# Linear attention ahead of a mixture of experts: the attention loop rewritten with row and column tiles on TensorE, scores one chunk ahead, and loads that don't wait for stores

## The chip, the cores and the metric

The kernel runs on one core of a Trainium2 chip. It is one program with five engines: TensorE (PE, its weight loads are shown as PEld), VectorE (DVE), ScalarE (ACT), GpSimd (POOL) and SyncE (SP), which here only issues DMAs. The metric is the device time of one execution in microseconds (us), lower is better.

## What is computed

```python
for t in range(S):                                   # B, H, S, D = 2, 8, 768, 48
    kt, vt, rt = (k[:, :, t], v[:, :, t], r[:, :, t])
    cur = np.einsum('bhd,bhe->bhde', u[None] * kt, vt)
    y[:, :, t] = np.einsum('bhd,bhde->bhe', rt, state + cur)
    state = w[None, :, :, None] * state + np.einsum('bhd,bhe->bhde', kt, vt)
x = y as (1536 tokens, 384)
logits = x @ w_gate                                  # 8 experts, the best one takes the token
...                                                  # each expert keeps its first 384 tokens
out[i] = gate[i] * (relu(x[i] @ w1[e]) @ w2[e])
g = relu(out @ w_in) ** 2                            # d_ff 2048
result = g @ w_out
```

Here w is a decay per head and feature, u a bonus that the token gives to itself.

## The kernel before, in words

**Stages.** First the attention, in chunks of 128 tokens; then routing (which token goes to which expert) and the gather of the tokens' rows from DRAM; then eight experts with four pieces of weights each and an MLP over the tokens in three blocks of 512, with eight pieces each. The experts and the MLP use f32r matmuls on values that are split into a high and a low part (whi and wlo, xshi and xslo), which the change does not touch.

**The attention loop.** There are 12 chunks: 6 along the sequence for each of 2 batches, taken in turn, so that chunk n belongs to batch n % 2. The loop runs 3 times over 4 slots (`for u in range(SLOTS)`), and slot u has its own input buffers. Heads lie in pairs (g of 4): the even head's 48 features stand in partitions 0 to 47, the odd head's in 64 to 111 (ROWS = 112). Within a chunk the recurrence is three products: scores of the chunk's keys against its queries, masked so that only earlier tokens count; the queries against the state before the chunk; and the bonus of each token with itself. Powers of w come from a table T made at the start (L746 to L769); keys and queries are scaled with them.

- SP (L279 to L312): loads feat (queries and keys by feature), vT, rk (queries and keys by token) and vx for the first four chunks and two pieces of expert weights; then for each chunk n it waits for x of n, issues its store to DRAM, waits until that store has landed (`x_stored`, L306), and only then issues the four loads of chunk n + 4. The wait for the landing is there because the buffers of slot u are reused.
- POOL (L360 to L373): scales keys (L364) and queries (L365), then khat (keys by token, for the state, L371) and ru (queries times u by token, L373).
- ACT (L620 to L641): copies the scaled keys into Kb, where each head has zeros in the other head's rows; copies v times gate from PSUM into vx; copies vx into vb, again with zeros; and scales the state St into Sd in four instructions (L640).
- PE (L414 to L447): v times gate (L421), scores (L427), the new state's product (L435), then for each head pair the state's part (L443) and the masked scores' part (L445) of y. Each f32 matmul is carried out as two instructions, a transpose as one. All of them use the whole array, 128 or 112 stationary columns.
- DVE (L784 to L811): masks the scores in two halves (L790), multiplies ru by the keys (L794) and sums over features (csum, L795), multiplies vx by csum (cv, L797), adds cv to y (x_sb L800 and heads_l L801), adds the new product to the state (L806, two instructions) and sums the heads' parts of the gate logits into L (L809).

DVE, ACT and PE take the chunks in order, and each of them does a chunk's steps in the order of the list. y of chunk n needs the masked scores and the state after chunk n - 2.

**After the loop.** DVE works out from L which token goes where (from L830), PE counts (L452 to L461), POOL gathers the first expert's rows from DRAM (L384), PE turns them (L513) and the first hidden matmuls begin (L477). Pieces 2 and 3 of the weights are issued behind the last loads of the loop, pieces 4 to 7 as soon as the lo part of pieces 0 to 3 has been split off (L313 to L315).

Of the kernel before, what the change touches and what calls it, by code (L numbers as in the profile page):

```python
# [20 lines left out]
P = 128  # L21
F32 = mybir.dt.float32
# [4 lines left out]
ALU = mybir.AluOpType  # L27
# [29 lines left out]
CONSTS = 10  # L57
SLOTS = 4

def build(nc, feat_d, vT_d, rk_d, vx_d, w_d, u_d, wg_d, wts_d, xd, out):
    with ExitStack() as ctx:
# [47 lines left out]
        with ExitStack() as a:  # L110
            feat = [sb(f"feat{u}", [P, 2, G * C], F32, a) for u in range(SLOTS)]
            rk = [sb(f"rk{u}", [P, 2, DM], F32, a) for u in range(SLOTS)]
            vx = [sb(f"vx{u}", [P, H, DX], F32, a) for u in range(SLOTS)]
            vT = [sb(f"vT{u}", [P, KT, C], F32, a) for u in range(SLOTS)]
            Rd = [sb(f"Rd{u}", [P, G * C], F32, a) for u in range(SLOTS)]
            Kb = [sb(f"Kb{u}", [P, G, 2, C], F32, a) for u in range(2)]
            vb = [sb(f"vb{u}", [P, G, 2, 2 * DX], F32, a) for u in range(2)]
            khat = [sb(f"khat{u}", [P, G, P], F32, a) for u in range(SLOTS)]
            ru = [sb(f"ru{u}", [P, DM], F32, a) for u in range(SLOTS)]
            x_sb = [sb(f"x_sb{u}", [P, DM], F32, a) for u in range(SLOTS)]  # L120
            am = sb("am", [P, 2, G * C], F32, a)
            csum = sb("csum", [P, H], F32, a)
            cv = sb("cv", [P, H, DX], F32, a)
            heads_l = sb("heads_l", [P, H, E], F32, a)
            St = [sb(f"St{b}", [P, G, 2 * DX], F32, a) for b in range(B)]
            Sd = sb("Sd", [P, G, 2 * DX], F32, a)
            T = sb("T", [P, G, 256], F32, a)
            Tk = sb("Tk", [P, G, C], F32, a)
            Tr = sb("Tr", [P, G, C], F32, a)
            iw = sb("iw", [P, G], F32, a)  # L130
            wcol = sb("wcol", [P, G], F32, a)
            tokw = sb("tokw", [P, G, P], F32, a)
            ub = sb("ub", [P, DM], F32, a)
# [12 lines left out]
        bank = [ctx.enter_context(nc.psum_tensor(f"bank{j}", [P, 512], F32)) for j in range(8)]  # L146
        ps_a0, ps_a1, ps_y, ps_kv, ps_x, ps_pos, ps_tab, ps_tab2 = bank
        ps_a = [ps_a0, ps_a1]
# [23 lines left out]
        tr_ready = sem("tr_ready")  # L172
        tokw_psum = sem("tokw_psum")
        tokw_ready = sem("tokw_ready")

        k_decayed = sem("k_decayed")
        r_decayed = sem("r_decayed")
        kb_cleared = sem("kb_cleared")
        kb_ready = sem("kb_ready")
        sd_ready = sem("sd_ready")  # L180
        khat_ready = sem("khat_ready")
        ru_ready = sem("ru_ready")
        khat_cleared = sem("khat_cleared")
        vb_cleared = sem("vb_cleared")
        vb_ready = sem("vb_ready")
        scored = sem("scored")
        masked = sem("masked")
        kv_done = sem("kv_done")
# [870 lines left out]
```

## Time and profile before

| | us |
|---|---|
| median of 3 runs (lowest, highest) | 481.53 (480.67, 483.12) |
| the profiled execution | 486.22 |
| its span, first to last instruction | 484.5 |
| PE busy, whole span | 437.6 (90%) |
| DVE busy | 300.9 (62%) |
| ACT busy | 219.9 (45%) |
| POOL busy | 112.2 (23%) |

The profile is of one execution. Busy time of PE is modelled from instructions that overlap one another, so a busy PE isn't PE at its peak; where the text needs the price of a matmul it takes the step from one to the next out of the chain of waits. L12 is line 12 of the kernel. In an instruction's shape, 128\*112 is the stationary operand, and 128x112 behind it the moving one. "<-" behind an idle time names what ended it.

### The profile page before, as it was taken

The numbers are of one execution on the slowest core, as the hardware profiler recorded it, in microseconds if no ns is written. First come the engines' busy times: TensorE is split into PE (matmuls) and PEld (weight loads), VectorE is DVE, ScalarE is ACT, GpSimd is POOL, SyncE is SP. The second block draws the span as 40 slices with busy tenths as digits, with TensorE's granted clock in tenths as the row PEclk, the third lists the DMA queues.
The fourth block names the chain that finished last, engine by engine and source line by source line (L and its number), as shares of the span: only waits on it lengthen the run. The fifth ranks groups of instructions, "written<-read, shape, count | busy, mean of one in ns | idle before, by whom it ended". The sixth has DMA issues, their size and how long they took to land.

```text
span 484.5 us, 8560 instructions
## 1 busy us (share of the span) xinstructions
PE 437.6 (90%) x2922; PEld 412.2 (85%) x2923; DVE 300.9 (62%) x494; ACT 219.9 (45%) x382; POOL 112.2 (23%) x110
## 2 busy tenths in 40 slices
PE   3998988723979999999999999999999999999993
PEld 3997978612979999999999989899898989899892
DVE  8797989883564677577676385454645545454431
ACT  3453544511454555565565364444544444444320
POOL 6855765528620220210000000000300000300003
PEclk9998999965898999999999999999999999999997
DMA  8966676504593555654555523232431313400001
GB/s 205 277 235 199 188 222 197 210 22 171 169 391 107 193 185 171 218 171 179 195 159 170 197 66 129 67 102 95 126 134 65 130 65 129 133 0 0 1 0 65
DMA packets 20990, 69.50 MB, mean 143 GB/s; under 512 B 3353, under 2 KB 9770, under 8 KB 20961
## 3 DMA queue, kind: packets, MB, share of 16 engines
q1 hardware_dynamic: 18656, 64.40, 41.2%
q0 software_dynamic: 2304, 4.73, 2.7%
q8 instruction: 17, 0.28, 0.2%
q14 instruction: 13, 0.10, 0.1%
HBM read 64.39 MB, written 7.08 MB: 148 GB/s over the span
## 4 chain that ended last, share of the span: by engine, by line
PE 76%; DVE 13%; issue 6%; DMA 2%; DVEq 1%; POOL 0%; ACT 0%; POOLq 0%; ACTq 0%
PE bank L477 34%; PE bank L496 21%; PE bank L486 14%; DVE cv L797 3%; DVE ru L794 2%; PE bank L445 2%; DMA xg<-attention_out,gidx 2%; PE bank L468 1%; DVE am L790 1%; DVE St L806 1%; PE bank L427 1%; PE bank L443 1%; DVE csum L795 1%; PE bank L435 1%; DVE L L809 1%
## 5 line engine op out<-in xcount | busy, mean ns | idle before, releaser
L908 DVE TENSOR_TENSOR wlo<-raw,whi 128x1536 fp32r<-128x1536 f32 x56 | 98.4, 1758 | 100.3 <-ACT whi L615 100.3
L615 ACT ACTIVATE whi<-raw 128x1536 fp32r<-128x1536 f32 x56 | 83.2, 1488 | 87.5 <-PE bank L496 47.1
L397 POOL DMA_INDIRECT out<-osb,oidx x12 | 13.0, 1084 | 247.7 <-ACT osb L730 245.3
L496 PE MATMUL bank<-whi,hhi 128*128 128x384 f32 x192 | 64.9, 338 | 0.5 <-DVE hlo L927 0.5
L496 PE MATMUL bank<-wlo,hhi 128*128 128x384 f32 x192 | 64.8, 338 | 0.0
L496 PE MATMUL bank<-whi,hlo 128*128 128x384 f32 x192 | 64.8, 338 | 0.0
L477 PE MATMUL bank<-xshi,whi 128*128 128x256 f32 x192 | 57.0, 297 | 5.0 <-issue 3.3
L477 PE MATMUL bank<-yhi,whi 128*128 (+1 forms) x144 | 57.1, 396 | 0.0
L477 PE MATMUL bank<-yhi,wlo 128*128 (+1 forms) x144 | 57.0, 396 | 0.0
L477 PE MATMUL bank<-ylo,whi 128*128 (+1 forms) x144 | 56.6, 393 | 0.0
L486 PE MATMUL bank<-hhi,whi 128*128 128x256 f32 x192 | 55.9, 291 | 0.0
L477 PE MATMUL bank<-xshi,wlo 128*128 128x256 f32 x192 | 55.7, 290 | 0.0
L477 PE MATMUL bank<-xslo,whi 128*128 128x256 f32 x192 | 55.6, 289 | 0.0
L486 PE MATMUL bank<-hhi,wlo 128*128 128x256 f32 x192 | 54.2, 282 | 0.0
L486 PE MATMUL bank<-hlo,whi 128*128 128x256 f32 x192 | 53.9, 281 | 0.0
L669 ACT ACTIVATE rl<-bank 128x512 f32<-128x512 f32 x48 | 28.6, 600 | 54.6 <-PE bank L477 51.1
L923 DVE TENSOR_TENSOR sq<-rl 128x512 f32<-128x512 f32 x48 | 32.9, 690 | 30.1 <-ACT rl L669 30.1
L384 POOL DMA_INDIRECT xg<-attention_out,gidx x24 | 27.7, 1156 | 91.4 <-PE bank L468 71.3
L477 PEld LDWEIGHTS bank<-xshi,whi 128*128 128x128 f32 x192 | 37.9, 197 | 6.3 <-issue 3.7
L477 PEld LDWEIGHTS bank<-xslo,whi 128*128 128x128 f32 x192 | 38.2, 199 | 0.0
L496 PEld LDWEIGHTS bank<-whi,hhi 128*128 128x128 f32 x192 | 36.1, 188 | 1.9 <-issue 0.9
L477 PEld LDWEIGHTS bank<-xshi,wlo 128*128 128x128 f32 x192 | 37.7, 196 | 0.0
(155 smaller groups left out, 848.8 us busy)
## 6 DMA issues: line engine op xcount, KB each, us to landing
raw<-in_wts SPq DMA_DIRECT2D x56, 768.0 KB, 4.7
feat<-in_feat SPq DMA_DIRECT2D x12, 448.0 KB, 4.0
rk<-in_rk SPq DMA_DIRECT2D x12, 384.0 KB, 4.6
vx<-in_vx SPq DMA_DIRECT2D x12, 224.0 KB, 5.1
vT<-in_vT SPq DMA_DIRECT2D x12, 192.0 KB, 3.8
attention_out<-x_sb SPq DMA_DIRECT2D x12, 192.0 KB, 4.9
out<-rl SPq DMA_DIRECT2D x12, 192.0 KB
xg<-attention_out,gidx POOLq DMA_INDIRECT x24, 5.9
```

The source lines that it names most:

```text
L384: nc.gpsimd.indirect_dma_start(out=xg[e % 2][:, q, :], out_offset=None, in_=xd[:, :], in_offset=bass.IndirectOffsetOnAxis(ap=gidx[:, e * C ...
L397: nc.gpsimd.indirect_dma_start(out=out[:, :], out_offset=bass.IndirectOffsetOnAxis(ap=oidx[:, t:t + 1], axis=0), in_=osb[:, t, :], in_offs ...
L445: mm = pe.matmul(pair, am[:, g // 2, (2 * (g % 2) + o) * C:(2 * (g % 2) + o + 1) * C], vb[u % 2][:, g, o, :], start=False, stop=(o == 1))
L477: mm = pe.matmul(banks[ft][:, 0:width], w[:, r, cols], x(k), start=(k == 0 and step == 0), stop=(k == KT - 1 and step == 2))
L486: mm = pe.matmul(ps_e[dt][:, 0:width], w[:, r, cols], x[:, par, ft, 0:width], start=(q == 0 and ft == 0 and step == 0), stop=(q == EQ - 1 ...
L496: mm = pe.matmul(ps_o[tt][:, 0:DM], x[:, par, ft, tt * P:(tt + 1) * P], w[:, r, cols], start=(v == 0 and ft == 0 and step == 0), stop=(v = ...
L615: return nc.scalar.activation(dst, src, ACT.Copy)
L669: nc.scalar.activation(rl[:, ft, :], banks[ft][:, :], ACT.Relu).then_inc(h_relu, 1)
L794: after(v.tensor_tensor(ru[u][:, :], ru[u][:, :], rk[u][:, 1, :], ALU.mult))
L797: after(v.tensor_tensor(cv[:, :, :], vx[u][:, :, :], csum[:, :].unsqueeze(2).to_broadcast([P, H, DX]), ALU.mult))
L908: v.tensor_tensor(wlo[:, r, :], raw[:, r, :], whi[:, r, :].bitcast(F32), ALU.subtract).then_inc(w_lo, 1)
L923: v.tensor_tensor(sq[:, ft, :], rl[:, ft, :], rl[:, ft, :], ALU.mult).then_inc(h_sq, 1)
```

## The change

- SP: chunk 0 is loaded ahead of the gate weights. The load of chunk n + 4 waits for x of chunk n to be summed, then the store of chunk n is issued once ACT has copied it; nothing waits for a landing but ACT, before it writes the same x_sb buffer four chunks later. rk is no longer loaded. Weight pieces 0 to 3 are issued behind the stores of chunks 1, 3, 5 and 7; pieces 4 to 7 wait for the three first gathers.
- POOL: keys and queries are scaled in place; khat and ru go.
- PE: `scores(n + 1)` (v times gate, the keys turned by four transposes, the scores) runs before the rest of chunk n. The stationary operand is cut in halves of 64 columns (column tiles, at output partitions 0 and 64) for v times gate, csum, the state's product and y; scores and the state's part of y use 48 rows at partition 0 or 64 (row tiles), so that no zeros are needed. The bonus is a matmul of prod (queries times keys) with a two-column operand (csum). Matmuls with 56 moving columns take the place of 112 wide ones.
- ACT: copies the turned keys to kT and the v times gate part to vx, scales the state in four instructions, copies x to x_sb. Kb, vb and Sd go.
- DVE: prod, one mask instruction 1024 wide, cv (its factor csum now in PSUM), Sn (the state's sum), yx (y plus cv, both parts in one), L. ru, csum, heads_l go.
- The loop of PE and DVE runs twice and the last four chunks are written out; those of ACT and SP are written out wholly. The power table is half as long, some constants and clearings go, and v and the gate weights lie in another head order.

```diff
...
+            sp.dma_start(ucol[0:ROWS, :], u_d).then_inc(in_u, 16)
             sp.dma_start(wg[:, :, :], wg_d).then_inc(in_wg, 16)
-            for u in range(SLOTS):
+            for u in range(1, SLOTS):
                 load_chunk(0, u)
-                if u == 0:
-                    sp.dma_start(ub[:, :], u_d.partition_broadcast(P)).then_inc(in_u, 16)
-            load_weights(0, 0)
-            load_weights(1, 1)
-            with sp.Fori(1, NC_ // 2) as i:
+            for i in range(1, NC_ // 2 + 1):
                 for u in range(SLOTS):
-                    sp.wait_ge(x_ready, 4 * (i - 1) + u + 2)
+                    n = 4 * (i - 1) + u
+                    if i < NC_ // 2:
+                        sp.wait_ge(x_ready, n + 2)
+                        load_chunk(i, u)
+                    sp.wait_ge(x_copied, n + 3)
                     store_x(i - 1, u)
-                    sp.wait_ge(x_stored[u], 16 * i)
-                    load_chunk(i, u)
-            load_weights(2, 2)
-            load_weights(3, 3)
-            for u in range(SLOTS):
-                sp.wait_ge(x_ready, NT - SLOTS + u + 2)
-                store_x(NC_ // 2 - 1, u)
+                    if n % 2 and n < 2 * RING:
+                        load_weights(n // 2, n // 2)
+            for q in range(CT):
+                sp.wait_ge(first_gathered[q], 16)
...
-                    keys = chunk_view(feat[u][0:ROWS, 1, :])
-                    nc.gpsimd.tensor_tensor(keys, keys, Tk[0:ROWS, :, :], ALU.mult).then_inc(k_decayed, 1)
-                    nc.gpsimd.tensor_tensor(chunk_view(Rd[u][0:ROWS, :]), chunk_view(feat[u][0:ROWS, 0, :]),
+                    nc.gpsimd.tensor_tensor(chunk_view(feat[u][0:ROWS, 1, :]), chunk_view(feat[u][0:ROWS, 1, :]),
+                                            Tk[0:ROWS, :, :], ALU.mult).then_inc(k_decayed, 1)
+                    nc.gpsimd.tensor_tensor(chunk_view(feat[u][0:ROWS, 0, :]), chunk_view(feat[u][0:ROWS, 0, :]),
                                             T[0:ROWS, :, 0:C], ALU.mult).then_inc(r_decayed, 1)
-                    pool.wait_ge(in_tok[u], 32 * (i + 1))
-                    pool.wait_ge(tokw_ready, 1)
-                    pool.wait_ge(khat_cleared, SLOTS if u else 1)
-                    pool.wait_ge(in_u, 16)
-                    nc.gpsimd.tensor_tensor(gapped(khat[u][:, :, :]), pairs(rk[u][:, 1, :]),
-                                            gapped(tokw[:, :, :]), ALU.mult).then_inc(khat_ready, 1)
-                    nc.gpsimd.tensor_tensor(ru[u][:, :], rk[u][:, 0, :], ub[:, :], ALU.mult).then_inc(ru_ready, 1)
...
+            def scores(i, u):
+
+                n = 4 * i + u
+                pe.wait_ge(in_vT[u], 16 * (i + 1))
+                for k in range(KT):
+                    for half in halves:
+                        pe.matmul(ps_vwg[half, 0:H * E], vT[u][:, k, half], wg[:, k, :], start=(k == 0), stop=(k == KT - 1))
+                pe.wait_ge(k_decayed, n + 1)
+                for g in range(G):
+                    mm = pe.transpose(ps_kT[:, g * ROWS:(g + 1) * ROWS], feat[u][0:ROWS, 1, g * C:(g + 1) * C], ident[0:ROWS, 0:ROWS])
+                mm.then_inc(turned, 1)
+                pe.wait_ge(r_decayed, n + 1)
+                for g in range(G):
+                    for o, rows in enumerate(heads):
+                        mm = pe.matmul(score_banks[:, o, g * C:(g + 1) * C], feat[u][rows, 1, g * C:(g + 1) * C],
+                                       feat[u][rows, 0, g * C:(g + 1) * C], start=True, stop=True)
+                mm.then_inc(scored, 1)
+
+            def attend(i, u, last):
+
+                n, p, b = 4 * i + u, u % 2, u % 2
+                pe.wait_ge(vx_ready, n + 1)
+                if not last:
+                    pe.wait_ge(masked, n + 1)
+                    if u < SLOTS - 1:
+                        scores(i, u + 1)
+                    else:
+                        scores(i + 1, 0)
+                pe.wait_ge(prod_ready, n + 1)
+                pe.wait_ge(summed, n + 1)
+                for g in range(G):
+                    for half in halves:
+                        pe.matmul(ps_csum[half, 0:H].rearrange("p (o g) -> p g o", o=2)[:, g, :],
+                                  prod[p][0:ROWS, g * C + half.start:g * C + half.stop], bonus[0:ROWS, g, :], start=True, stop=True)
+                pe.wait_ge(x_ready, n + 1)
+                pe.wait_ge(state_ready, 4 * n + 4)
+                for g in range(G):
+                    for o, width in enumerate((HALF, D)):
+                        mm = pe.matmul(ps_kv[ODD * o:ODD * o + width, g * DX:(g + 1) * DX], kT[p][:, g, ODD * o:ODD * o + width],
+                                       vx[u][:, o * G + g, :], start=True, stop=True)
+                mm.then_inc(kv_done, 1)
+                for g in range(G):
+                    pair = slice(g * DX, (g + 1) * DX)
+                    for half in halves:
+                        for o, rows in enumerate(heads):
+                            mm = pe.matmul(y_banks[half, o, pair], feat[u][rows, 0, g * C + half.start:g * C + half.stop],
+                                           St[b][rows, g, :], start=True, stop=False)
+                    if g == G - 1:
+                        mm.then_inc(state_read, 1)
+                    if g == 0:
+                        pe.wait_ge(masked, n + 1)
+                    for o in range(2):
+                        for half in halves:
+                            mm = pe.matmul(y_banks[half, o, pair], am[p][:, o * G + g, half], vx[u][:, o * G + g, :],
+                                           start=False, stop=True)
+                mm.then_inc(y_done, 1)
...
+            def columns(i, u):
+
+                n = 4 * i + u
+                act.wait_ge(turned, n + 1)
+                copy(kT[u % 2][:, :, :].rearrange("p g r -> p (g r)"), ps_kT[:, 0:G * ROWS]).then_inc(kT_ready, 1)
+                act.wait_ge(in_tok[u], 16 * (i + 1))
+                copy(vx[u][:, :, D:DX], ps_vwg[:, 0:H * E].rearrange("p (h e) -> p h e", h=H)).then_inc(vx_ready, 1)
+
+            def advance(i, u, last):
+
+                n, b = 4 * i + u, u % 2
+                if not last:
+                    if u < SLOTS - 1:
+                        columns(i, u + 1)
+                    else:
+                        columns(i + 1, 0)
+                act.wait_ge(summed, n + 2)
+                act.wait_ge(state_read, n + 1)
+                for g in range(G):
+                    nc.scalar.activation(St[b][0:ROWS, g, :], Sn[b][0:ROWS, g, :], ACT.Copy,
+                                         scale=T[0:ROWS, g, 129:130]).then_inc(state_ready, 1)
+                act.wait_ge(x_ready, n + 2)
+                if i:
+                    act.wait_ge(x_stored[u], 16 * i)
+                copy(x_sb[u][:, :].rearrange("p (g o d) -> p o g d", g=G, o=2),
+                     yx[u % 2][:, :, 0:D].rearrange("p (o g) d -> p o g d", o=2)).then_inc(x_copied, 1)
...
+            def weigh(i, u):
+
+                n, p = 4 * i + u, u % 2
+                dve.wait_ge(r_decayed, n + 1)
+                v.tensor_tensor(prod[p][w, :], feat[u][w, 0, :], feat[u][w, 1, :], ALU.mult).then_inc(prod_ready, 1)
+                dve.wait_ge(scored, n + 1)
+                v.tensor_tensor(am[p][:, :, :], score_banks[:, :, :].rearrange("p o (g s) -> p (o g) s", g=G),
+                                before[:, :].unsqueeze(1).to_broadcast([P, H, C]), ALU.mult).then_inc(masked, 1)
+
+            def collect(i, u, last):
+
+                n, p, b = 4 * i + u, u % 2, u % 2
+                if not last:
+                    if u < SLOTS - 1:
+                        weigh(i, u + 1)
+                    else:
+                        weigh(i + 1, 0)
+                dve.wait_ge(kv_done, n + 1)
+                after(v.tensor_tensor(cv[:, :, :], vx[u][:, :, :], ps_csum[:, 0:H].unsqueeze(2).to_broadcast([P, H, DX]), ALU.mult))
+                dve.wait_ge(state_ready, 4 * n + 4)
+                v.tensor_tensor(Sn[b][w, :, :], ps_kv[w, 0:G * DX].rearrange("p (g e) -> p g e", g=G), St[b][w, :, :],
+                                ALU.add).then_inc(summed, 1)
+                dve.wait_ge(y_done, n + 1)
+                dve.wait_ge(x_copied, n + 1)
+                v.tensor_tensor(yx[p][:, :, :].rearrange("p (o g) d -> p o (g d)", o=2), y_banks[:, :, 0:G * DX],
+                                cv[:, :, :].rearrange("p (o g) d -> p o (g d)", o=2), ALU.add).then_inc(x_ready, 1)
+                dve.wait_ge(x_ready, n + 2)
+                after(v.tensor_reduce(L[:, bass.ds(n, 1), :].rearrange("p a e -> p (a e)"),
+                                      yx[p][:, :, D:DX].rearrange("p h e -> p e h"), AX.X, ALU.add))
...
```

## Rows read from the trace of the kernel before

**Rows 1.** Stages: length; busy us of PE, PEld, DVE, ACT, POOL; clock, DMA, GB/s

```profile
...
20.00:32.00 12.00, 12.00 (x112) 12.00 (x111) 10.97 (x21) 6.51 (x19) 7.98 (x7) 1.00 0.79 258
32.00:98.00 66.00, 55.71 (x469) 53.73 (x467) 57.89 (x92) 30.83 (x78) 40.35 (x34) 0.97 0.65 206
...
```

**Rows 2.** Chain that ended last: start, us; the first scores, then one chunk

```profile
10.51 3.52 PE bank L427 x16
...
46.41 0.63 PE bank L421 x6
47.04 1.84 PE bank L427 x16
48.88 0.79 PE bank L435 x8
...
49.88 0.45 PE bank L445 x4
...
```

**Rows 3.** Waits of the queue of SP: total us, times, longest

```profile
SPq L281 <- DMA attention_out<-x_sb: 41.0, 8, 9.7
...
```

**Rows 4.** Instructions in time, SP's queue: start, us, what

```profile
...
36.59 0.33 SPq L281 DMA_DIRECT2D feat<-in_feat  x1
...
38.74 0.36 SPq L289 DMA_DIRECT2D attention_out<-x_sb  x1
...
```

**Rows 5.** DMA issues of the page: times, KB each, median us to landing

```profile
feat<-in_feat SPq DMA_DIRECT2D x12, 448.0 KB, 4.0
...
attention_out<-x_sb SPq DMA_DIRECT2D x12, 192.0 KB, 4.9
...
```

**Rows 6.** Groups by shape, 0 to 125 us: busy, mean ns | idle before

```profile
...
L364 POOL TENSOR_TENSOR feat<-feat,Tk 112x512 f32<-112x512 f32 x12 | 15.7, 1305 | 23.0 <-DMA feat<-in_feat 23.0
L790 DVE TENSOR_TENSOR am<-bank,before 128x512 f32<-128x512 f32 x24 | 15.6, 687 | 3.4 <-DVE L L809 1.1 <-PE bank L427 1.0
...
```

**Rows 7.** Instructions in time, 51 to 60 us, DVE and POOL

```profile
...
51.56 0.63 DVE L797 TENSOR_TENSOR cv<-vx,csum 128x448 f32<-128x448 f32 x1
...
57.82 2.83 DVE L797 TENSOR_TENSOR cv<-vx,csum 128x448 f32<-128x448 f32 x1
...
59.16 1.00 POOL L373 TENSOR_TENSOR ru<-rk,ub 128x384 f32<-128x384 f32 x1
...
```

**Rows 8.** Instructions in time: POOL's first, a quiet ru, weights behind routing

```profile
...
7.22 1.27 POOL L364 TENSOR_TENSOR feat<-feat,Tk 112x512 f32<-112x512 f32 x1 [1.98 <-DMA feat<-in_feat]
...
93.16 0.55 DVE L794 TENSOR_TENSOR ru<-ru,rk 128x384 f32<-128x384 f32 x1
...
107.46 2.97 SPq L292 DMA_DIRECT2D raw<-in_wts  x2
...
```

**Rows 9.** The same chain: gaps of DVE, then routing, gather and a turn

```profile
38.65 0.42 issue
...
39.83 0.40 DVE St L806
...
97.87 0.26 DVE r_mx L830
...
99.56 0.55 PE bank L454 x12
...
105.24 0.68 issue
...
108.83 7.42 DMA xg<-attention_out,gidx
...
149.07 0.33 PE bank L468 x3
...
```

**Rows 10.** Groups by shape, PE: 128 or 112 stationary columns, 112 moving

```profile
L445 PE MATMUL bank<-vb,am 128*128 128x112 f32 x192 | 30.4, 283 | 0.0
...
L435 PE MATMUL bank<-vx,khat 128*112 128x112 f32 x96 | 12.4, 276 | 7.0 <-DVE St L806 7.0
...
```

More of the change, by code:

```diff
@@ L57, with build @@
 CONSTS = 10
+HALF = P // 2
 SLOTS = 4
-def build(nc, feat_d, vT_d, rk_d, vx_d, w_d, u_d, wg_d, wts_d, xd, out):
+def build(nc, feat_d, vT_d, vx_d, w_d, u_d, wg_d, wts_d, xd, out):
     with ExitStack() as ctx:
@@ L188, in build @@
         kv_done = sem("kv_done")
+        summed = sem("summed")
+        state_read = sem("state_read")
         state_ready = sem("state_ready")
@@ L191, in build @@
         x_ready = sem("x_ready")
-        vwg_psum = sem("vwg_psum")
-        vx_ready = sem("vx_ready")
+        x_copied = sem("x_copied")
         shifted = sem("shifted")
@@ L404, in _ @@
         def _(pe):
+            halves = [slice(0, HALF), slice(HALF, P)]
+            heads = [slice(0, D), slice(ODD, ROWS)]
+            def scores(i, u):
[14 more added lines that the diff above has]
+                mm.then_inc(scored, 1)
@@ L449, in _ @@
+                    attend(i, u, False)
+            for u in range(SLOTS):
+                attend(NC_ // 2 - 1, u, u == SLOTS - 1)
             pe.wait_ge(oh_ready, 1)
@@ L643, in split_hi @@
+            columns(0, 0)
+            for i in range(NC_ // 2):
+                for u in range(SLOTS):
+                    advance(i, u, 4 * i + u == NT - 1)
             def split_hi(m, r, turns):
@@ L746, in _ @@
             v.memset(T[w, :, 64:65], 1.0)
[L747 to L748 removed]
+            v.memset(oh[:, :, :], 0.0)
             dve.wait_ge(in_w, 16)
@@ L775, in _ @@
-            v.memset(x_sb[SLOTS - 1][:, :], 0.0).then_inc(x_ready, 1)
-            for u in range(1, SLOTS):
-                v.memset(khat[u][:, :, :], 0.0).then_inc(khat_cleared, 1)
+            v.tensor_copy(Tk[w, :, :], T[w, :, 127::-1]).then_inc(table_ready, 1)
+            v.tensor_tensor(T[w, :, 129], T[w, :, 128], T[w, :, 128], ALU.mult)
+            after(v.memset(bonus[w, :, :], 0.0))
+            dve.wait_ge(in_u, 16)
+            for o in range(2):
+                rows = slice(ODD * o, ODD * o + D)
+                v.tensor_tensor(bonus[rows, :, o], ucol[rows, :], wcol[rows, :], ALU.mult).then_inc(bonus_ready, 1)
@@ new lines, in _ @@
+            v.memset(Sn[0][:, :, :], 0.0).then_inc(summed, 1)
+            for b in range(B):
+                v.memset(St[b][:, :, :], 0.0).then_inc(state_ready, 4)
+            v.memset(start[:, :], 0.0).then_inc(x_ready, 1)
+            v.memset(kept[:, :], 0.0).then_inc(x_copied, 2)
+            dve.wait_ge(consts, 2)
+            def weigh(i, u):
[5 more added lines that the diff above has]
+                                before[:, :].unsqueeze(1).to_broadcast([P, H, C]), ALU.mult).then_inc(masked, 1)
@@ L778, in _ @@
+            weigh(0, 0)
+            with dve.Fori(0, NC_ // 2 - 1) as i:
+                steps.enter(i, 2 * SLOTS)
+                for u in range(SLOTS):
+                    collect(i, u, False)
+                steps.leave(NC_ // 2 - 1)
+            for u in range(SLOTS):
+                collect(NC_ // 2 - 1, u, u == SLOTS - 1)
             v.memset(gout[:, :], 0.0).then_inc(y_ready, 1)
```

176 lines of the change are left out of this document (35 added, 141 removed).

## The prediction

> **What bounds the kernel now.** I read the stages first. The attention loop fills the span from 8.5 to 98 us, then come some 21 us of routing and gather, then 365 us of expert and MLP matmuls, where the page shows PE busy nine tenths or more in nearly every slice. Only the first stage is rewritten, so the question is what ends one chunk (12 chunks, one batch's 128 tokens each) and how the next stage starts. In the loop the stages have two paces. From 20 to 32 us PE is busy for all 12 of 12 us, and the steps of a chunk add up to 0.63 + 1.84 + 0.79 + 4 x 0.67 = 5.9 us [rows 1, 2]; from 32 to 98 us PE is busy 84% and DVE 88% [rows 1]. The reader should not stop at the engine with the largest share: the queue that issues DMAs shows why the pace falls. SP waits 41.0 us in 8 waits for a store of x_sb to land, before it may issue the next loads [rows 3]. Its cycle is four loads, from 36.59 to 38.74 2.15 us, then a store, which lands 4.9 us after its issue [rows 4, 5], and some 0.2 us of waking: 7.3 us a chunk. Behind it POOL waits for feat, 23.0 us in all [rows 6], and everything follows. The bunching has a second effect: cv on DVE, with two inputs in SBUF, takes 0.63 us in one chunk and 2.83 us in the next, where it ends (60.65) only after POOL's operation from 59.16 to 60.16 has ended [rows 7]. So three limits stand close together: SP's order 7.3 us, DVE with its waits some 7 us, PE 5.9 us.
>
> **SP.** The loads of chunk n+4 no longer wait for the store of chunk n to land; they need that x(n) is summed. One load of four (rk, 384 KB) goes. SP then issues three loads and a store a chunk at 0.54 us each, 2.2 us [rows 4]; the 768 KB weight pieces move from before the loop to behind chunks 1, 3, 5 and 7, 0.5 us each. Queued behind SP's wait for x_copied are the next loads; that copy comes only some 0.7 us after x is summed (an ACT copy of 0.5, a wait of 0.2, by ACT's tokw copy of 0.54 us), so this costs nothing. Is a load early enough? From x(n) to the matmuls that need chunk n+4: 0.5 us issue, 4.0 us landing [rows 5], 2.6 us on POOL (2 x 1.305 [rows 6]), 7.1 us; two chunks at 6 us, less 0.8, give 11.2. It stays hidden down to a chunk of 4 us. Volume: 448+192+224+192 KB and, in the first eight, 384 KB of weights, 1.44 MB in 6 us, 240 GB/s, where 258 GB/s were moved from 20 to 32 us at a DMA share of 0.79, so up to some 325 [rows 1]. This is the thinnest cover of the three; if it tears, feat is late as now.
>
> **DVE.** Gone per chunk: ru, csum, heads_l and the second St; cv takes its factor from PSUM, so it has one SBUF input. Left or new: prod 512 wide, 0.55 x 512/384 = 0.73 from the ru at 93.16, when POOL is quiet [rows 8]; am 1024 wide, two of 0.687 less an overlap, 1.29 [rows 6]; cv 0.63 [rows 7]; Sn 0.40 as one St [rows 9]; yx 448 wide, as cv, 0.63; L 0.27 as before: 3.95 us. A gap between dependent steps is up to 0.42 us [rows 9]; six at half of that give 1.2. That is 5.15, and up to 2.2 more if prod meets POOL as cv did; I take 5.3.
>
> **ACT and POOL.** ACT is busy 30.83 of 66 us [rows 1], 3.4 us a chunk; it loses Kb and vb (four copies) and gets kT and the copy of x (two, 0.5 each), so it does less than now. POOL keeps 2.6 us and loses khat and ru. Neither is near 6 us.
>
> **PE, the term that decides.** Every f32 matmul is two instructions, a transpose one. Before, a chunk has 6+16+8+8+16 = 54. After: 12 for v times gate, 4 transposes, 16 scores, 16 csum, 16 kv, 64 for y (16 state and 16 am matmuls), 128 in all. What does one cost? The step is 0.45/4 = 0.112 us with 128 stationary columns and 112 moving, 0.115 with 128 and 128, 0.105 with 128 and 64, but 0.79/8 = 0.099 with 112 and 112 [rows 2, 10]. The moving width hardly counts and the stationary one does (0.099/0.112 = 0.88, 112/128 = 0.875). So a half of 64 columns should cost 0.056. Whether two tiles in different halves run side by side no row shows, since before has none. Upper end, not at all: 108 x 0.056 + 4 x 0.11 (0.33 for 3 [rows 9]) + 16 x 0.112 = 8.3 us. Lower end, all in pairs: 108 x 0.028 + 0.44 + 0.9 = 4.4 us. A chunk may thus cost PE less or more than the present 5.9. I take 6.0, a little below the middle (6.35), because the order written in the change alternates halves from matmul to matmul, for which only the shortest seen step speaks as a floor: bf16 steps of 0.55/12 = 0.046 us [rows 9]. 108 x 0.042 + 0.44 + 0.9 = 5.9, and 0.1 for waits.
> The rule most in favour is in the Trainium skill, "TensorE: Matmul & The Clock Gate", Part 3 (packing small matmuls): matmuls of different row or column tiles run at once. By that alone the sum is that of the lower end; no run here shows it yet.
>
> **What orders a chunk after.** PE does scores(n+1), then csum, kv and y of n. am(n+1) is made while kv and y(n) run (2.4 us of DVE work beside over 4 us of PE work), and kv(n) waits for yx(n-1), some 0.9 us after y(n-1), which lies beside scores (1.9 us). So the masks leave the path, and the longer engine's sum sets the pace: PE 6.0, DVE next at 5.3. Two waits are new. ACT waits for the store of four chunks ago before it copies x; the next kT and vx stand behind it, but that store has some 20 us for its 4.9. PE waits for the mask of n before scores(n+1), one PSUM pair only, with all of chunk n behind it; the mask is made 2.5 us after the scores, beside kv and y of n-1, so it is ready.
>
> **The start and the rest.** The first feat load is issued one place earlier, about half a microsecond, as wg moves behind chunk 0. POOL began at 7.22 [rows 8]; so keys are ready at 8.0 and queries at 9.3. Scores at the start ran at half pace (3.52 us for 16 against 1.84 [rows 2]): 1.8 us in pairs, and am with its wait 1.5: 12.6, I say 12.8. Of twelve chunks the last has no scores to make (v times gate 0.5, 0.44, 0.9). A slow first chunk 1.5, the last yx and L 1.3. L is complete at 12.8 + 72 - 1.85 + 1.5 + 1.3 = 85.8 us, against 97.87 [rows 9]: 12.1 us gained. The constants, tokw and zeroing that go lay beside POOL's wait: nothing.
> From L to gidx the code is the same. The stores: the last x is copied 0.5 us later and lands 4.9 us after [rows 5], while the indices take 7.4 us (97.87 to 105.24 [rows 9]): hidden, 2 us to spare. The gathers: SP now holds back the weight pieces 4 to 6 until the first three have landed; before, two pieces went out from 107.46 on [rows 8], beside the 7.42 us for which the chain waits for the gather [rows 9]. POOL's own work of issuing fills part of that time, so I give it 1.0 us, between 0 and 2. The held pieces then come some 9 us later, 7 to 9 us for 2.3 MB, while the first four pieces are in SBUF and are worked through first; I cost it at nothing, and at up to 3 us if that cover is short. The 365 us behind are not touched.
>
> **Sum.** 12.1 + 1.0 = 13.1 us. The profiled execution took 486.22 us (span 484.5), so 473.1; it was 4.7 us above the median of the runs, which I subtract: 468.4 us.
>
> **The rivals.**
> - Tiles pair fully and DVE is the bound. PE 4.4, DVE 5.3: 0.7 us x 12 = 8.4 less, 460.0 us. For: the order of the matmuls. Against: nothing below 0.046 a step is seen.
> - Slower: each change between full, row-split and column-split use empties the array. A matmul lasts 0.283 us [rows 10] while the next starts after 0.112 [rows 2]; the tail is 0.17. Per chunk the form changes 3 times before csum and 8 times in kv and y, where state and am alternate by head pair: 11 x 0.17 = 1.9 us, x 12 = 22.4, 490.8 us. It decides from about 0.10 us a change, where a chunk passes 7.1 us. Before has no such change, so the trace is silent. Beside it: the Trainium skill, "TensorEngine Tiling (Array Packing)", Key Properties, says that a change of tiling mode drains the engine.
> - Slower as well: halves don't pair at all, 8.3 us, 27.6 more, 496 us.
> - It moves nothing: prod, the one operation with two SBUF inputs, meets POOL each time as cv did (2.2 us longer), DVE needs 7.3, the pace of now. Gain left from the start alone: 12 x 1.3 = 15.6 less gain, 484.0 us. For: POOL has work all the time once loads run free. Against: POOL is busy 2.55 of 6 us only. Loads that come late through the added weight traffic would give the same time.
>
> **How the numbers follow.** Forecast 0.46, pairs fully 0.22, array emptied 0.13 (half of the price in a third of these cases, near 480), not paired 0.05, nothing moved 0.14. A measurement of this kernel can tell about 0.5%, 2.4 us. Faster: 0.46 + 0.22 and some of the nothing-moved and half-price cases, 0.75; same 0.08; slower 0.17. Range 456 to 491: down past the DVE bound by the doubt of the start and gather terms (4 us), up to the emptied array; only the unpaired case and tails are out.
>
> **What would show it.** Right: SP has no wait for the landing of a store; POOL's waits for feat are short; from 20 us on PE is the busy engine and chunks come every 6 us; the groups for csum, kv and y have a spacing near 0.04 us; L complete near 86 us. Wrong: a y stage of over 3.5 us a chunk (tiles not paired, or gaps at each change of form); prod over 1.5 us; feat landing after 6 us; a granted clock of a half in the loop; or a gap at the first weight pieces behind the gather, which would show as a wait for wlo after 119 us.

## The result and the profile after

The changed kernel takes 507.88 us (median of 4 runs, 506.29 to 509.43), the kernel before, run beside it, 482.32 us (480.67 to 483.82). The ratio is 1.0546, with a 95% interval from 1.0493 to 1.0599: 25.6 us slower. The profiled execution has a span of 504.6 us, against 484.5.

The loop ends later and the rest is shorter. L is complete (the start of r_mx) at 124.75 us, before at 97.87 [rows 9]: 26.9 us later. From there to the end it is 379.9 us, before 386.6: 6.8 us less. The sum is the 20.1 us between the spans.

First the stretches: length, then busy us of PE, PEld, DVE, ACT and POOL, the granted clock, the DMA share and GB/s (the counterpart of [rows 1]).

```profile
...
20.00:50.00 30.00, 30.00 (x408) 25.38 (x408) 11.49 (x18) 6.66 (x21) 7.49 (x6) 1.00 0.43 136
50.00:80.00 30.00, 30.00 (x410) 25.49 (x404) 12.01 (x19) 7.70 (x25) 7.48 (x6) 1.00 0.49 161
...
```

PE is busy in all of the time, up to 110 us too, and nothing else is near it: DVE 40%, the DMAs under half. So nothing waits that matters. The chain that ended last shows one chunk (start, us, what), the counterpart of [rows 2]:

```profile
60.29 0.65 PE bank L391 x12
60.95 0.94 PE bank L394 x4
61.89 2.01 PE score_banks L399 x16
63.90 0.95 PE bank L417 x16
64.85 0.94 PE bank L423 x14
65.78 0.41 PE y_banks L430 x8
66.19 0.61 PE y_banks L438 x8
...
```

The two causes of waiting in the kernel before are gone. SP has no wait for a landed store left (41.0 us in [rows 3]). POOL's wait for feat has grown, from 23.0 [rows 6] to 59.3 us, against what the prediction named as a sign of being right, and it costs nothing: it is idle time of an engine that is ahead. Waits of 20 to 110 us (engine, line, waited for: total us, times, longest), then SP's:

```profile
POOL feat L346 <- DMA feat<-in_feat: 59.3, 8, 9.7
DVE yx L809 <- PE y_banks L438: 29.5, 10, 3.0
...
SPq L267 <- DVE yx L809: 68.0, 8, 14.9
SPq L274 <- ACT x_sb L617: 31.9, 4, 9.2
```

### The profile page after: what moved, and what is told of

Read it like the earlier page. It is cut to its first block, busy times and chain, and to the rows that moved or that the text cites. A ratio compares the mean times of both kernels' runs of the same rounds, so it can differ in the third digit from the quotient of the medians.

```text
span 504.6 us, 9950 instructions
## 1 busy us (share of the span) xinstructions
PE 471.9 (94%) x3806; PEld 431.0 (85%) x3807; DVE 268.4 (53%) x442; ACT 205.5 (41%) x357; POOL 84.2 (17%) x85
## 4 chain that ended last, share of the span: by engine, by line
PE 90%; DVE 3%; issue 2%; DMA 2%; DVEq 1%; POOL 0%; SPq 0%; ACT 0%; POOLq 0%; ACTq 0%
PE score_banks L479 17%; PE bank L479 15%; PE y_banks L498 10%; PE bank L498 10%; PE y_banks L488 9%; PE y_banks L438 6%; PE score_banks L399 5%; PE bank L488 4%; PE y_banks L430 4%; PE bank L423 2%; PE bank L394 2%; PE bank L417 2%; PE bank L391 2%; PE bank L470 1%; DMA xg<-attention_out,gidx 1%
## 5 line engine op out<-in xcount | busy, mean ns | idle before, releaser
L488 PE MATMUL y_banks<-hhi,whi 128*128 128x256 f32 x128 | 37.8, 296 | 0.0
L488 PE MATMUL y_banks<-hhi,wlo 128*128 128x256 f32 x128 | 36.1, 282 | 0.0
L488 PE MATMUL y_banks<-hlo,whi 128*128 128x256 f32 x128 | 36.0, 281 | 0.0
L498 PE MATMUL y_banks<-whi,hhi 128*128 128x384 f32 x96 | 32.5, 338 | 0.5 <-DVE hlo L942 0.5
L438 PE MATMUL y_banks<-vx,am 128*64 128x56 f32 x384 | 32.6, 323 | 0.0
L498 PE MATMUL y_banks<-whi,hlo 128*128 128x384 f32 x96 | 32.4, 338 | 0.0
L498 PE MATMUL y_banks<-wlo,hhi 128*128 128x384 f32 x96 | 32.4, 338 | 0.0
L498 PE MATMUL bank<-whi,hhi 128*128 128x384 f32 x96 | 32.4, 338 | 0.0
L498 PE MATMUL bank<-wlo,hhi 128*128 128x384 f32 x96 | 32.4, 338 | 0.0
L498 PE MATMUL bank<-whi,hlo 128*128 128x384 f32 x96 | 32.4, 338 | 0.0
```

What stands on the lines that cost most here:

```text
L438: mm = pe.matmul(y_banks[half, o, pair], am[p][:, o * G + g, half], vx[u][:, o * G + g, :], start=False, stop=True)
L488: mm = pe.matmul(ps_e[dt][:, 0:width], w[:, r, cols], x[:, par, ft, 0:width], start=(q == 0 and ft == 0 and step == 0), stop=(q == EQ - 1 ...
L498: mm = pe.matmul(ps_o[tt][:, 0:DM], x[:, par, ft, tt * P:(tt + 1) * P], w[:, r, cols], start=(v == 0 and ft == 0 and step == 0), stop=(v = ...
```

## The experiments

Two theories stood after the result. One: changes between full array, row tiles and column tiles are dear, and half matmuls hardly pair. Two: they pair, and the pattern of matmuls keeps the clock at its lower level. Wherever a diff is not against the kernel after, the text says so.

**e1: the freed loads by themselves** (diff against the kernel before).

```diff
                     store_x(i - 1, u)
-                    sp.wait_ge(x_stored[u], 16 * i)
                     load_chunk(i, u)
...
                     dve.wait_ge(y_done, n + 1)
+                    dve.wait_ge(x_stored[u], 16 * i + 1)
```

> The kernel before with one part of the change: the loads of chunk n+4 no longer wait for the store of chunk n to land (VectorE waits for that before it writes the same x_sb buffer). If the order of SP's queue set the 7.3 us pace from 32 to 98 us, nine chunks fall to the next bound, TensorE's 5.9 us or VectorE's 6.4 us with its gaps: 0.8 to 1.3 us each, 7 to 12 us in all, 470 to 475 us. If VectorE held behind GpSimd (cv up to 2.83 us) set the pace by itself, the time stays within 2 us of 482.

477.15 us (474.16 to 479.28, 10 runs), ratio 0.9893 (0.9856 to 0.9931). The gain is real and is some 5 us, less than the 7 to 12 expected. SP no longer waits for a landed store, and PE takes its place as the bound: it is on the chain for nearly all of the loop, and its chunks follow at its own pace.

```profile
...
56.23 2.83 DVE cv L798
...
66.45 0.63 PE bank L420 x6
67.08 1.84 PE bank L426 x16
...
72.66 0.63 PE bank L420 x6
...
```

From 66.45 us a chunk begins every 5.9 to 6.2 us, the 5.9 that PE's steps add up to. cv clashes with POOL less often than before: cv takes 2.8 us once in the twelve chunks (56.23), four times in the kernel before. That one clash is dear. The two chunks from 50.42 to 66.45 us take 16.0 us, two others 11.9: PE waits 1.8 us for the state, and its next steps are at the lower level of the clock (0.86 us at 62.37 for four of am, 0.45 elsewhere). In these two traces L is complete 5.2 us earlier (92.70, 97.87 before), though e1's first chunk began 1.9 us later. A further gain needs fewer PE steps.

**e2: the same matmuls of y, in two groups**: all 16 state matmuls, then all 16 am matmuls. Per chunk 2 changes of form in y in place of 8.

```diff
-                                           St[b][rows, g, :], start=True, stop=False)
-                    if g == G - 1:
-                        mm.then_inc(state_read, 1)
-                    if g == 0:
-                        pe.wait_ge(masked, n + 1)
+                                           St[b][rows, g, :], start=(g == 0), stop=False)
+                mm.then_inc(state_read, 1)
+                pe.wait_ge(masked, n + 1)
+                for g in range(G):
...
-                                           start=False, stop=True)
+                                           start=False, stop=(g == G - 1))
```

> The changed kernel, y of a chunk made in two groups: all 16 matmuls with the state first, then all 16 with the masked scores, so that the array's form changes twice and not eight times in y. Theory A (each change of form costs some 0.18 us, read from the extra gap of 0.14 between the last start before it and the first behind it and 0.04 in the next step): 6 x 0.18 x 12 = 13 us less, 495 us, and y takes 3.0 us a chunk where it takes 4.08. Theory B (halves of 64 columns run one after another at 0.05 to 0.06 us, a change of form costs nothing): no change, 508 us.

457.54 us (456.65 to 459.2), ratio 0.9502 (0.9425 to 0.958): 50.3 us less than the kernel after, by an order. No theory had given that much. With the order, the start and stop flags of the accumulation change too. Its chain, from the second chunk on:

```profile
...
13.91 2.01 PE score_banks L399 x16
15.93 0.95 PE bank L417 x16
16.87 0.93 PE bank L423 x14
17.81 1.05 PE y_banks L430 x32
18.86 1.86 PE y_banks L438 x32
20.72 0.36 PE bank L391 x12
21.07 0.54 PE bank L394 x4
21.61 1.09 PE score_banks L399 x16
22.70 0.56 PE bank L417 x16
23.27 0.51 PE bank L423 x14
23.77 0.62 PE y_banks L430 x32
24.39 1.08 PE y_banks L438 x32
```

Up to 20.7 us each step is that of the kernel after (2.01, 0.95, 0.93). Then the same lines take 1.09, 0.56 and 0.51: the clock is at its upper level, and a chunk takes 4.7 us. In the kernel after, PE works without a gap from 12.2 us on and this never comes. Both parts of the 4.8 us between the two chunks can be read here. Grouping alone saves, at the lower level, 4.08 - 2.91 = 1.17 us a chunk; the clock gives the other 3.7 us.

**e3 and e3b: do halves pair?** e3 leaves out the am matmuls of the second half, e3b makes am's matmuls 128 columns wide, uncut.

```diff
                     for o in range(2):
-                        for half in halves:
-                            mm = pe.matmul(y_banks[half, o, pair], am[p][:, o * G + g, half], vx[u][:, o * G + g, :],
-                                           start=False, stop=True)
+                        mm = pe.matmul(y_banks[:, o, pair], am[p][:, o * G + g, :], vx[u][:, o * G + g, :],
+                                       start=False, stop=True)
```

> The changed kernel without the second column half of the masked scores' matmuls in y (left out: tokens 64 to 127 of each chunk get no part from earlier tokens of the chunk); 16 of the 32 instructions go. Theory A (two tiles start 7 ns apart and run side by side, and a tile's own step is 0.107 us, weight load and stream one after the other): the other half takes as long alone, the time stays at 508 within 2 us. Theory B (one after another): 16 x 0.053 us less a chunk, 10 us, 498 us.

> The changed kernel with the masked scores' matmuls in y uncut: 8 matmuls with 128 stationary columns in place of 16 with 64. By theory A a pair of halves costs what one full matmul costs (0.107 us an instruction), and the number of changes of form stays: 508 us within 2 us. If tiles were a gain of any size over full width, this would be slower: at no gain from hiding the load (0.16 us a step) by 0.05 x 16 x 12 = 10 us.

e3: 505.94 us (505.64 to 506.41), the kernel after is 507.88. Leaving out every second tile saves next to nothing, so the second tile ran beside the first. Its chain has four am steps of one half where the kernel after has eight of both, in 0.61 us:

```profile
65.99 0.60 PE y_banks L438 x4
```

e3b: 528.5 us (528.47 to 528.84), 20.6 us more. In its chain four uncut am steps stand for eight halves:

```profile
...
64.04 0.41 PE y_banks L430 x8
64.45 1.03 PE y_banks L437 x4
...
```

1.03 us in place of 0.61, for the same product. The two halves together cost less than one uncut matmul, and one half alone as much as both: they pair. The Trainium skill, "TensorE: Matmul & The Clock Gate", Part 3, says that matmuls on different column tiles run at once; the trace agrees.

**e5 and e12: the kernel after with 22 full matmuls ahead of the first scores.** Both are the same kernel, run on two chips.

```diff
             pe.wait_ge(consts, 1)
+            for j in range(22):
+                pe.matmul(ps_csum[:, 128:256], ident[:, :], ident[:, :], start=True, stop=True)
             pe.wait_ge(in_wg, 16)
```

> The changed kernel with 22 full-width f32 matmuls on TensorE ahead of the first scores (into unused PSUM columns), where it waits for its first inputs; they take some 9 us at the low clock and may delay the start by 2 to 4 us. Theory C (new): the 507.9 us come from TensorE staying at its 1.2 GHz level through the whole loop; the same column-half step is 0.107 us there and 0.058 us in the run with y grouped. C1 (once raised, the clock stays): a chunk falls from 9.56 to about 5.5 us, the time to 460 to 468 us. C2 (this loop's pattern of work doesn't hold the upper level): the clock rises in the burst and falls back within a few chunks, 500 to 512 us. The older reading (a tile's load and stream don't overlap, changes of form cost 0.18 us each) gives 508 to 512 us and steps of 0.107 us throughout.

> The changed kernel with 22 full-width matmuls ahead of the first scores once more, six executions: the first time one of four took 466 us and three 510 us. If the loop at the upper clock is kept or lost by chance of its phase, both values come again and nothing between; if the one was an outlier of that chip, all are near 510 us.

Ten executions, two values and nothing between: 466.32 and 465.97 us, and eight from 508.1 to 510.92. The mean granted clock is 0.965 in the two and 0.859 to 0.863 in the eight. The loop's order of matmuls is that of the kernel after in all ten. Two of them are shown. Here is one of 466 us, a chunk at 52.55 us:

```profile
52.55 0.36 PE bank L391 x12
52.91 0.53 PE bank L394 x4
53.44 1.09 PE score_banks L399 x16
54.53 0.56 PE bank L417 x16
55.10 0.51 PE bank L423 x14
55.60 0.27 PE y_banks L430 x8
55.87 0.38 PE y_banks L438 x8
...
```

5.6 us a chunk in place of 9.57. In this execution the clock was up before the first scores (1.12 us at 9.53) and was still up behind the pause for the first mask (10.65 to 12.14 us). And here is one of the others, by its stretches and its chain:

```profile
...
6.00:12.00 6.00, 5.76 (x58) 5.24 (x57) 3.64 (x9) 0.66 (x2) 5.38 (x5) 1.00 1.05 300
12.00:18.00 6.00, 4.72 (x64) 4.29 (x64) 3.91 (x3) 0.66 (x2) 4.63 (x4) 0.69 0.45 122
18.00:24.00 6.00, 6.00 (x87) 4.77 (x83) 2.34 (x5) 1.58 (x6) 0.00 (x0) 0.50 0.01 3
...
50.00:70.00 20.00, 20.00 (x276) 17.00 (x276) 7.66 (x12) 4.74 (x16) 5.00 (x4) 0.50 0.45 147
...
10.67 1.12 PE score_banks L399 x16
...
11.81 1.24 DVE am L793
...
14.38 2.01 PE score_banks L399 x16
...
```

The burst raised the clock (scores 1.12 us). Then PE had to wait for the first mask, from 11.79 to 13.28 us, and the next scores are at 2.01 us again. The pause is as long as in the execution of 466 us, which kept the clock (1.5 us in both). What differs ahead of it is when the clock rose: the burst's 44 instructions took 7.9 us here and 6.77 there, where their steps get shorter at some 5 us in place of 7. One trace of each kind is too few to call that the cause. From 18 us on the granted clock is 0.50, PE is busy for all of the time, and it doesn't rise again in the loop. The scores beside that 0.50 take 2.01 us, as in the kernel after: this is what shows that the kernel after ran at 1.2 GHz. It is also the main result of the study. In these runs this order of matmuls keeps the upper level where it has it inside the loop and doesn't reach it from below, so the same program has two paces.

**e6: is PE not loaded enough?** The kernel after with one full matmul of 448 columns more in each chunk.

```diff
                 pe.wait_ge(summed, n + 1)
+                pe.matmul(ps_csum[:, 64:512], ident[:, :], vx[u][:, :, :].rearrange("p h d -> p (h d)"), start=True, stop=True)
```

> The changed kernel with one idle full-width f32 matmul more in each chunk (128 stationary, 448 moving columns, into unused PSUM columns): pure extra work, 1.5 us a chunk at the low clock and 0.75 us at the upper one. If the clock's level is set by how densely the array is used, the extra matmul can raise it: a chunk of 5.5 + 0.75 us, 12 x 3.3 us less, near 470 us. If the clock isn't what holds the loop, the time rises by 12 x 1.5 = 18 us, to 526 us.

529.24 us (528.15 to 530.22), 21.4 us more than the kernel after.

```profile
59.75 2.01 PE score_banks L399 x16
61.76 1.79 PE bank L415 x2
...
```

12 x 1.79 = 21.5 us: the added matmul costs its own time at the lower level and the clock stays. e3b says the same, with full matmuls in place of the halves (its scores take 2.01 us too). Added work of a full array, with the 8 changes of form kept, doesn't raise it.

**e7: e2 with the loads behind the landed store**, as in the kernel before (diff against e2).

```diff
-                    if i < NC_ // 2:
-                        sp.wait_ge(x_ready, n + 2)
-                        load_chunk(i, u)
                     sp.wait_ge(x_copied, n + 3)
                     store_x(i - 1, u)
+                    if i < NC_ // 2:
+                        sp.wait_ge(x_stored[u], 16 * i)
+                        load_chunk(i, u)
```

> The kernel with y grouped, its loads put behind the landing of the store of the same slot again, as before the change. SP's cycle is then three loads (1.4 to 1.6 us), a store and its landing (3.9 to 4.9 us) and the copy of x: 6 to 7 us a chunk against 5.0 now, for eight chunks: 8 to 16 us more, 466 to 473 us. If the freed loads bring nothing once TensorE is fast, 458 us.

473.76 us (471.93 to 475.9), 16.2 us more than e2. The wait, and two stretches:

```profile
SPq L267 <- DMA attention_out<-x_sb: 34.6, 8, 7.5
...
30.00:40.00 10.00, 9.70 (x267) 8.62 (x260) 7.41 (x13) 4.21 (x14) 4.29 (x4) 1.00 0.60 189
40.00:50.00 10.00, 5.86 (x96) 5.01 (x90) 2.90 (x6) 2.22 (x7) 2.49 (x2) 0.65 0.64 187
...
```

So the freed loads are worth 16 us behind a PE of 4.7 us a chunk, and 5 us in the kernel before, where PE's 5.9 us a chunk was next. A part of the 16 us is again the clock: where PE has to wait for a load, between 40 and 50 us, it falls, 0.65 in the mean, and it is 0.67 from 50 to 60 us.

**e8 and e10: e2 with full matmuls ahead**, 16 in e8; 24 in e10, which also loads ucol first (diff of e8 against e2).

```diff
             pe.wait_ge(consts, 1)
+            for j in range(16):
+                pe.matmul(ps_csum[:, 128:256], ident[:, :], ident[:, :], start=True, stop=True)
```

> The kernel with y grouped and 16 full-width f32 matmuls ahead of the first scores. There the steps are at the low level until about 20 us. If the clock rises by 12 to 15 us in place of 20, the first two chunks take 5 us and not 9: 3 to 7 us less, 451 to 455 us, less what the burst delays the start.

> The kernel with y grouped, 24 matmuls ahead of the first scores (in place of 16, so that no pause follows the burst) and u's column loaded ahead of chunk 0, since its landing held the first prod. With 16 matmuls the clock rose at 6 us and fell again from 13 to 20 us. If it now stays up, the second chunk takes 4.7 us in place of 8: 450 to 453 us. If the pause for the mask of chunk 0 is enough to lose it, 454 to 456 us.

e8: 455.31 us (453.47 to 461.43), ratio 0.9425 (0.9366 to 0.9484), the lowest median of all. e10: 461.44 us (456.74 to 469.03), ratio 0.9562 (0.9497 to 0.9627). Its interval overlaps that of e2 (0.9425 to 0.958), so it is no better than e2 without a burst, and not shown to be worse. In e10's chain:

```profile
10.53 1.12 PE score_banks L399 x16
...
14.99 2.01 PE score_banks L399 x16
...
23.41 1.09 PE score_banks L399 x16
```

The burst raised the clock, the wait for the first mask lost it, as in e12, and it came back at 23.4 us, later than in e2 (20.7). What a burst ahead of a wait gains can be lost in the wait. In e8 too it is lost by the second chunk and back at 19.9 us, 0.8 us earlier than in e2. The difference of e8 and e2, 2.2 us, is inside the spread of their runs.

**e9: y in two parts of two head pairs**, 4 changes in y, between e2 (2) and the kernel after (8) (diff against e2).

```diff
-                for g in range(G):
+                for part in ((0, 1), (2, 3)):
+                    for g in part:
```

> The changed kernel with y in two parts (two head pairs' state matmuls, their masked scores', then the other two pairs): four changes of form in y, where the changed kernel has eight and the grouped one two. Each change costs 0.20 us at the low clock and 0.15 us at the upper one (y 4.08 against 2.90, and 2.58 against 1.70 us, over six changes). If the clock stays low: 4 x 0.20 x 12 = 9.5 us less, 498 us. If it rises as in the grouped kernel: a chunk of some 5.0 us, 456 to 461 us. It tells on which side a half-way pattern falls.

460.37 us (458.96 to 463.36), ratio 0.9588 (0.9536 to 0.9639). The clock rises, at some 24 us, later than in e2. At the upper level:

```profile
...
56.13 0.39 PE y_banks L431 x16
56.51 0.61 PE y_banks L441 x16
...
```

y takes 2 x (0.38 + 0.61) = 1.98 us with 4 changes, 1.70 with 2 (e2) and 4 x (0.27 + 0.38) = 2.60 with 8 (e5). That is 0.15 us a change, and at the lower level (4.08 - 2.91)/6 = 0.20 us. The Trainium skill, "TensorEngine Tiling (Array Packing)", Key Properties, says that a change of tiling mode drains the array; the trace agrees that a change costs time and gives it this price.

**e11: e2 without SP's hold on the weight pieces behind the gather** (diff against e2).

```diff
-            for q in range(CT):
-                sp.wait_ge(first_gathered[q], 16)
```

> The kernel with y grouped, without SP's wait for the first three gathers before weight pieces 4 to 6. If those pieces' traffic lengthened the gather before the change (7.42 us of waiting there, 4.05 after), 3 to 4 us more: 461 us. If the gather is bound by GpSimd's own issuing, 457 to 458 us.

456.4 us (455.71 to 456.88), ratio 0.9505 (0.9465 to 0.9545), against e2's 457.54: no difference that these runs can tell. The chain waits 5.95 us for the gather in e11, 4.11 us in e2 and 4.05 us in the kernel after, 7.42 us before [rows 9]:

```profile
85.31 4.11 DMA xg<-attention_out,gidx
```

```profile
83.95 5.95 DMA xg<-attention_out,gidx
```

The first line is e2's chain, the second e11's. By one trace of each, the hold makes the wait for the gather 1.8 us shorter; the whole time shows no gain from it.

## Why the prediction was wrong

The forecast was 468.4 us, in a range of 456 to 491; it took 507.9.

**The step that failed** is the clock. The working costed the start at half pace, gave "a slow first chunk 1.5", and from there took every step at the pace of [rows 2] at the upper level. That the clock would rise after a chunk of unbroken PE work was assumed from the kernel before, where it did. In the kernel after it doesn't rise in twelve chunks. The price: 9.57 - 5.62 = 3.95 us a chunk, some 43 us over the loop; 507.9 against the 466 us that the same loop takes in e5 and e12 where it keeps the upper level. The text did name "a granted clock of a half in the loop" as what would make it wrong, but gave it no chance of its own and no price, though [rows 2] had both levels to price it: twice 6 us.

**With the clock at the upper level the forecast comes near, in part by luck.** PE was put at 6.0 us a chunk, it measures 5.62 in e5, and the total, 468.4, compares with 466.3 and 466.0. But L is complete at 80.16 us in e5, where the working had 85.8, and the 4.7 us subtracted at the end, by which the profiled execution of the kernel before was slow, made up for most of that. Inside a chunk two errors cancel: halves were priced too high, and the changes of form, 8 x 0.15 = 1.2 us a chunk in y alone, were put at nothing. The terms:
- Pairing. The working took 0.042 us for an instruction on a half, bounded by 0.028 and 0.056. It measures at or near the lower bound where no form changes: e2's am, 32 in 1.08 us, 0.034 each; its state matmuls, 32 in 0.62, 0.019, below it (each uses half of the rows as well as half of the columns). The floor of 0.046 us a step that I took from [rows 9] was no floor for tiles. e2's chunk of 4.7 us is near the 4.4 of the rival "tiles pair fully".
- The emptied array. The rival's 0.17 us a change measures 0.15 at the upper level, 0.20 at the lower. So its price was right; that an emptied array is what takes the time is argued, no trace shows the array itself. It stood as an alternative to pairing when both hold: 4.7 us with 2 changes in y, 5.6 with 8. Its 490.8 us came out of adding it to steps of 0.042 us, where paired ones take 0.034.
- Transposes. 0.53 us for four at the upper level, 0.44 predicted.
- Scores. 1.09 us for 16 as row tiles, 0.9 predicted.

**DVE was not the bound.** The working gave it 5.3 us. In the kernel after it waits 29.5 us for PE. Even in e2, with a chunk of 4.7 us, PE's steps follow one another without a gap in the rows shown. The terms were close: am 1.225 us (1.29), prod 0.788 (0.73), yx 0.625 (0.63), Sn 0.39 (0.40); what was too large was the 1.2 us of gaps between them. In the kernel after prod hardly meets POOL (0.69 us from the third chunk on). At e2's pace it does in three chunks of twelve (1.72 us at 26.68, 1.59 and 1.08), and PE doesn't wait for it, so "it moves nothing" is out.

**SP's order was the bound**, as argued: without it, 41.0 us of waits are gone [rows 3], and put back (e7) it costs 16.2 us. By itself in the old kernel it is worth only 5 us (e1), because PE's 5.9 us a chunk is next, the third of the close limits of the first part; DVE with its waits was put at some 7 us, and e1's chunks of 5.9 us show that it needs less when cv doesn't clash. The cover of the loads, which the prediction called the thinnest of the three and good down to a chunk of 4 us, is at its end at 4.7: in e2 the chain waits 7.68 us for feat to land (from 50.14 us), and PE is idle for 0.9 us between 50 and 70.

**The gather** gained 3.4 us, predicted 1.0, outside the 0 to 2. The hold is the cause of some 1.8 of it (e11), and it is no gain for the whole. **The weight pieces that come late** cost nothing that can be seen: the stall of 2.81 us at 142.49 in the chain of the kernel before is 0.89 at 148.17 now. Of the 6.8 us that the part behind the loop got shorter, the gather explains 3.4 and this stall 1.9; the one-hot matmuls cost 0.5 more (L456, 1.04 us for twelve, at the lower level, against 0.55 [rows 9]). A further 1.6 is the clock again, which was at its lower level behind the stall of the kernel before:

```profile
145.30 3.77 PE bank L477 x18
```

The same eighteen take 2.16 us elsewhere. But how much of the 6.8 us is the change's can't be told from two traces: one execution differs from another there by some 4 us with the same code. In e1 the code of the kernel before takes 382.7 us from L on, in place of 386.6, and the code of the kernel after takes 379.9 us in the profiled execution, 383.0 in e12 and 384.4 in e5, with stalls of 2.1 and 2.2 us in the last two.

**Still open.** What in the pattern of the matmuls decides whether the clock rises. The runs say that 2 or 4 changes of form in y let it rise and 8 don't, and that more full matmuls beside the 8 don't help. Between these orders the count of changes, the time for which the array stands empty, how the halves follow one another and the start and stop flags of the accumulation vary together, and no run here takes them apart. What decides which executions of e5 and e12 keep the clock over the pause of the first mask is open too.

The version that beats both kernels is e2 (457.5 us), with e8 and e11 within its spread: the change is worth 25 us over the kernel before, if y is grouped.

## What to carry to other kernels

Price a loop of small or tiled matmuls at both levels of TensorE's clock and give the lower one a chance, even where PE is never idle; the rise in one order of matmuls is no evidence for another. Group matmuls by their form first: it saves the price of each change and can decide the clock. Read the clock from the steps of one line in both traces, not from the column alone.

## What the hardware showed that was not expected

- TensorE busy without a gap from 12 to 117 us and at 1.2 GHz throughout: 16 scores at 2.01 us, 1.09 at the upper level.
- One program with two times: 466 us twice, 508 to 511 us eight times, which differ, in the two traces at hand, in whether the clock, raised ahead of the loop, outlives a pause of 1.5 us.
- An order of the same 32 matmuls a chunk that is worth 50.3 us of 507.9, some 14 of them by the changes of form (12 x 1.17) and the rest by the clock.
- A change of form costs 0.15 us at the upper level and 0.20 at the lower; two instructions on column halves of 64 together take 0.61/4 = 0.15 us at the lower level, a share of a change included, where the one uncut instruction in their place takes 1.03/4 = 0.26.
